# A three-stage chain on one core: the first tile's four opening hidden products, and the place of one weight subtraction

## The chip, the cores and the metric

One NeuronCore of a Trainium2 chip runs the whole program. The metric is the time of one execution on the device, in microseconds (us), taken as the median of several runs. The engines are named as in the profile: PE (TensorE, matrix products), PEld (its weight loads), DVE (VectorE), ACT (ScalarE), POOL (GpSimd), SP (SyncE, which here only issues DMAs).

## The reference

```python
X = np.fft.fft(x, axis=1); X = np.fft.fft(X, axis=2); x = X.real      # x is 4 x 3072 x 256
x_prev = x shifted by one along the sequence (a zero row first)
xk = mu_k * x + (1.0 - mu_k) * x_prev
xr = mu_r * x + (1.0 - mu_r) * x_prev
k = np.maximum(xk @ w_k, 0.0)                                         # w_k 256 x 1024
v = k * k @ w_v                                                       # w_v 1024 x 256
r = 1.0 / (1.0 + np.exp(-(xr @ w_r)))                                 # w_r 256 x 256
x = r * v
# then: top-1 routing to 8 experts of capacity 384, in order of the tokens;
# each expert: y = relu(x @ w1) @ w2, scaled by the gate's probability, back to the token's row
```

## The kernel before

Each fp32 operand of a large product is split into a high part (rounded to fp32r) and a low part (the original minus the high part), and a product is the sum of three matmuls: high by high, high by low, low by high (function product, L290 to L298). The high parts are written by ACT as copies, the low parts by DVE or POOL as subtractions, and semaphores count them.

Work is done in tiles of 512 tokens, six to a batch of 3072. For a batch, the two Fourier transforms come as matmuls (step 1, step 2, step 3) that leave the transposed result in the tile xt. The first batch's transform has nothing beside it and is written out in the functions first_dft of each engine. Its last pieces are the sums of step 3 (DVE, L920), their mirror images (ACT, L697), and an edge row that goes out and back in by DMA (L473, L475).

Then tile 0 is prepared on DVE and ACT: difference (L924) and mix (L931) give xk_raw and xr_raw for each half h of the 256 channels, high_part (ACT, L736, counted by x_high) and low_part (DVE, L937, counted by mixed) split them. The halves are xk 0, xk 1, xr 0, xr 1 in this order. The difference of half 1 waits for the edge's DMA.

The hidden layer has eight blocks f of 128 columns. An up(n, f) is six matmuls (three for each half of the channels) into the bank hb[f % 2]; ACT takes its relu (hidden, L753, counted by hb_drained), DVE squares it (L1037), ACT makes the high part (L748) and DVE the low part (L1032), and down(n, f) multiplies by w_v into the two banks vb. Eight PSUM banks exist: hb is banks 0 and 1, vb banks 2 and 3, rb (the gate's products) banks 4 and 5, and banks 6 and 7 serve the routing.

In the first tile of a batch, first_ups (L1318 to L1332) runs blocks 0 and 1 together: the high by high and low by high matmuls of half 0 of both blocks (L1327), then the high by low ones (L1330), then the same for half 1, so that PE can begin while half 1 isn't there yet. For n = 0, before(n) then issues up(0, 2) and up(0, 3) (L1370, L1371), each of which waits until ACT has taken the relu of the block that held its bank. Then come the gate's twelve matmuls (gate_in), which wait for the low parts of xr, and for wr_split in tile 0; then up 4, up 5, down 0, up 6 and so on. Up to that place PE runs four warming matmuls (keep_warm, L374) after step 3.

The weights w_k, w_r, w_v are split during the first transform: ACT makes the high parts between its other work (L713, L715, L717) and POOL subtracts in this order: four pieces of wk (L601), wr (L603), then casts half of wv (L605), four quarters of wv (L608), and two small casts and a copy for the routing (L610 to L612). DVE's own order in first_dft is: pairs and outputs of step 1, outputs of step 2 (even_out, L911, L912), sums of step 3 (L920), difference and mix of tile 0.

The order of each engine's work is written out by hand; the functions walk, before, after and rest go through the tiles. Tiles go on until every expert is full, which the kernel reads at run time.

Of the kernel before, what the change touches and what calls it, by code (L numbers as in the profile page):

```python
# [18 lines left out]
P = 128  # L19
# [25 lines left out]
TILES = SEQ // TOK  # L45
# [8 lines left out]
CREDIT = 2  # L54
# [41 lines left out]
def build(nc, ins, out, cap):  # L96
# [104 lines left out]
    hb = banks[0:2]  # L201
# [166 lines left out]

    edge_bank = banks[6]

    def keep_warm_with(count, stationary, moving, bank=lb):

        for _ in range(count):
            done = nc.tensor.matmul(bank[0:stationary.shape[-1], 0:moving.shape[-1]], stationary, moving, start=True, stop=True)  # L374
        return done
# [84 lines left out]
    with ctx:  # L460
        with nc.Block("main") as block:
# [129 lines left out]
            @block.gpsimd  # L591
            def _(pool):
                nc.gpsimd.memset(warm[:, :], 0.0).then_inc(setup, 1)
                nc.gpsimd.memset(blank[:, 0:ROW - 1], 0.0).then_inc(setup, 1)
                nc.gpsimd.memset(blank[:, ROW - 1:ROW], FAR).then_inc(setup, 1)
                nc.gpsimd.memset(full[:, 0:2], 0).then_inc(routed, 2)
                pool.sem_inc(rows_free, 1)
                nc.gpsimd.memset(padded[:, :, :], 0.0)
                for i, (h, cols) in enumerate(WK_PIECES):
                    pool.wait_ge(wk_high, i + 1)  # L600
                    nc.gpsimd.tensor_tensor(wk[:, 1, h, cols], raw_wk[:, h, cols], wk[:, 0, h, cols].bitcast(fp32), ALU.subtract).then_inc(wk_split, 1)  # L601
                pool.wait_ge(wr_high, 1)
                nc.gpsimd.tensor_tensor(wr[:, 1, :, :], raw_wr[:, :, :], wr[:, 0, :, :].bitcast(fp32), ALU.subtract).then_inc(wr_split, 1)  # L603
                pool.wait_ge(wv_in, 16)
                nc.gpsimd.tensor_copy(wv[:, 0, WV_HALVES[1], :], raw_wv[:, WV_HALVES[1], :]).then_inc(wv_high, 1)  # L605
                pool.wait_ge(wv_high, len(WV_HALVES))
                for part in WV_QUARTERS:
                    nc.gpsimd.tensor_tensor(wv[:, 1, part, :], raw_wv[:, part, :], wv[:, 0, part, :].bitcast(fp32), ALU.subtract).then_inc(wv_split, 1)  # L608
                pool.wait_ge(consts_in, 16 * CONSTS)
                nc.gpsimd.tensor_copy(earlier[:, :], small[:, 0:P])  # L610
                nc.gpsimd.tensor_copy(ones[:, :], small[:, P:2 * P])
                nc.gpsimd.tensor_copy(token[:, :], token0).then_inc(tables, 1)  # L612
                pool.wait_ge(slots_blank, 16)

                def route(m):
                    if m > 0:
                        pool.wait_ge(scattered, 16 * GRP * m)
                        pool.sem_inc(rows_free, 1)
                    pool.wait_ge(row_copied, CREDIT + GRP * (m + 1))
                    pool.wait_ge(slots_ready, m + 1)  # L620
                    if may_be_full(m):
                        pool.wait_ge(first_rows_in, 16 * needed_at(m))
                    for g in range(GRP):
                        nc.gpsimd.indirect_dma_start(  # L624
                            out=slots_dram,
                            out_offset=bass.IndirectOffsetOnAxis(ap=slot[:, g:g + 1], axis=0),
                            in_=rows[:, g, :], in_offset=None,
                            bounds_check=SLOTS - 1, oob_is_err=False,
                        ).then_inc(scattered, 16)

                def before(n):
                    if n > 0:
                        route(n - 1)

                walk(pool, before, lambda n: None, lambda: route(NTILE - 1))

                for left in (pe_left, act_left, dve_left, sp_left):
                    pool.wait_ge(left, 1)
                pool.wait_ge(w_in[0], 16)
                for half in (slice(0, FT // 2), slice(FT // 2, FT)):  # L640
                    nc.gpsimd.tensor_copy(down_w[0][:, 0, half, :], raw_down[0][:, half, :]).then_inc(down0_high, 1)
                for k, half in enumerate((slice(0, FT // 2), slice(FT // 2, FT))):
                    pool.wait_ge(down0_high, k + 1)
                    nc.gpsimd.tensor_tensor(down_w[0][:, 1, half, :], raw_down[0][:, half, :], down_w[0][:, 0, half, :].bitcast(fp32),
                                            ALU.subtract).then_inc(down0_ready, 1)
                pool.wait_ge(out_zeroed, 16 * ZEROED)
                with pool.Fori(0, EXPERTS // 2) as turn_no:
                    for i in range(2):
                        e = 2 * turn_no + i
                        for j in range(SP):  # L650
                            pool.wait_ge(ye_ready, SP + e * SP + j + 1)
                            pool.sem_inc(waits_held, 1)
                            nc.gpsimd.indirect_dma_start(  # L653
                                out=out, out_offset=bass.IndirectOffsetOnAxis(ap=who[:, i, j:j + 1], axis=0),
                                in_=ye[:, i, j, :], in_offset=None,
                                bounds_check=NTOK - 1, oob_is_err=False,
                            ).then_inc(written[i], 16)
                for i in range(2):
                    pool.wait_ge(written[i], 16 * SP * EXPERTS // 2)

            @block.scalar
            def _(act):
# [87 lines left out]
                def hidden(n, f):  # L750
                    act.wait_ge(hb_full, n * FT + f + 1)
                    act.wait_ge(square_ready, n * FT + f + 1)
                    nc.scalar.activation(relu[:, f % 2, :], hb[f % 2][:, :], ACT.Relu).then_inc(hb_drained, 1)  # L753
                    if f > 0:
                        square_high(n, f - 1)

# [117 lines left out]
            def _(dve):  # L874
# [64 lines left out]
                def first_dft():  # L939
                    pair(0, 0)  # L940
                    pair(0, 1)
                    step1_out(0, first_pairs, 0)
                    pair(0, 2)
                    step1_out(0, first_pairs, 1)
                    pair(0, 3)
                    pair(0, 4)
                    step1_out(0, first_pairs, 2)
                    step1_out(0, first_pairs, 3)
                    step1_out(0, first_pairs, 4)
                    for i in range(len(TRIPLES)):  # L950
                        even_out(0, first_pairs, i)
                    for g in range(QUADS):
                        sums(0, first_quads, g)
                    dve.wait_ge(consts_in, 16 * CONSTS)
                    dve.wait_ge(s3_summed, DH * QUADS)
                    dve.wait_ge(near_mirrored, DH * QUADS)
                    difference(0, 0, 0)
                    mix(0, 0, 0)
                    dve.wait_ge(near_edge_in, 32)
                    difference(0, 1, 0)  # L960
                    low_part(0, 0)
                    mix(0, 1, 0)
                    mix(0, 2, 0)
                    low_part(1, 0)
                    mix(0, 3, 0)
                    low_part(2, 0)
                    low_part(3, 0)
                    nc.vector.tensor_scalar(next_slot[:, :], expert_no, float(cap), None, ALU.mult)
                    nc.vector.tensor_scalar(limit[:, :], expert_no, float(cap), float(cap), ALU.mult, ALU.add)
# [240 lines left out]
            def _(pe):  # L1210
# [107 lines left out]
                def first_ups(n):  # L1318

                    for h in range(DH):  # L1320
# [8 lines left out]
                        for f in range(2):  # L1329
                            done = mm(hb[f][:, :], wk[:, 0, h, f * P:(f + 1) * P], xk[:, 1, h, :], start=False, stop=h == 1)  # L1330
                            if h == 1:
                                done.then_inc(hb_full, 1)  # L1332

                def gate_in(n, h, kh):
                    cut = slice(h * P, (h + 1) * P)
                    done = product(pe, rb[h][:, :], [(wr[:, 0, kh, cut], wr[:, 1, kh, cut], xr[:, 0, kh, :], xr[:, 1, kh, :])],
# [4 lines left out]
                def down(n, f):  # L1341
                    pe.wait_ge(squared, CREDIT + n * FT + f + 1)
                    if f == 0:
                        pe.wait_ge(x3_done, DH * (n + 1))
                        pe.wait_ge(row_copied, CREDIT + GRP * n)
                        if n == 0:
                            pe.wait_ge(wv_split, len(WV_QUARTERS))
                    for h in range(DH):
                        cut = slice(h * P, (h + 1) * P)
# [8 lines left out]

                def before(n):
                    seq, stage = n // TILES + 1, stage_of(n)  # L1360
                    if n % TILES == 0:
                        first_ups(n)
                        if n > 0:
                            route_rows(n - 1)
                    else:
                        pe.wait_ge(mixed, len(MIXED) * n + DH + 1)
                        up(n, 0)
                        route_rows(n - 1)
                        up(n, 1)
                    if n == 0:  # L1370
                        up(n, 2)  # L1371
                        up(n, 3)
                    pe.wait_ge(mixed, len(MIXED) * (n + 1) + 1)
                    pe.wait_ge(gated, DH * (n + 1))
                    if n == 0:
# [163 lines left out]
```

## Time and profile before

| | us |
|---|---|
| median of 3 runs | 614.53 |
| lowest, highest | 614.29, 615.75 |
| the profiled execution, its own time | 614.96 |
| its span (first to last instruction) | 613.2 |
| busy in it: PE, DVE, ACT, POOL | 598.6, 449.3, 316.1, 104.2 |
| mean granted TensorE clock | 0.994 |

The 1.8 us between the profiled execution's time and its span lie around the instructions. In rows of a timeline, the first number is the start in us from the beginning of the span, the second is the length of the group, then come the engine, the line, what is written and read, the shape and the count; brackets at the end give the idle time of the engine before it and what ended that.

### The profile page before, as it was taken

To read this page: it belongs to the slowest core of one execution; us is meant where nothing else is said; L and a number is where in the kernel's file an instruction comes from. 1 tells how busy PE (TensorE), PEld (TensorE's weight loads), DVE (VectorE), ACT (ScalarE), POOL (GpSimd) and SP (SyncE) were. 2 spreads that over 40 slices of the span, in tenths; PEclk is the share of its full clock that TensorE was granted. 3 is DMA by queue.
4 is the path that set the end of the run, shared out by engine and by line. 5 is a ranking of instruction groups with operands and counts; after the bars stand their busy time and mean duration, and the time that the engine had idled before them with its cause. 6 is when DMAs were issued, how large, how long until landed. Compare 5 with 4: busy or idle time off the path is not lost.

```text
span 613.2 us, 10505 instructions
## 1 busy us (share of the span) xinstructions
PE 598.6 (98%) x3358; PEld 516.0 (84%) x3358; DVE 449.3 (73%) x1053; ACT 316.1 (52%) x668; POOL 104.2 (17%) x106
## 2 busy tenths in 40 slices
PE   8989999999999999999999999999998999999995
PEld 5958888888888888888888888788887999999995
DVE  4577888877776688889786767787873777766671
ACT  1664545454546564645454545554543565664550
POOL 0720302020202011202020202020206111011111
PEclk9999999999999999999999999999998999999998
DMA  8439935151510005301010100033105834455000
GB/s 306 150 94 222 378 114 191 67 176 52 182 52 23 2 8 178 107 5 43 22 37 1 34 1 3 29 120 118 30 1 178 303 130 140 156 190 182 34 26 26
DMA packets 42157, 62.99 MB, mean 103 GB/s; under 512 B 4582, under 2 KB 32055, under 8 KB 42108
## 3 DMA queue, kind: packets, MB, share of 16 engines
q1 hardware_dynamic: 38268, 55.88, 28.3%
q0 software_dynamic: 3840, 6.52, 3.0%
q8 instruction: 23, 0.38, 0.3%
q14 instruction: 26, 0.21, 0.1%
HBM read 39.90 MB, written 26.91 MB: 109 GB/s over the span
## 4 chain that ended last, share of the span: by engine, by line
PE 92%; DVE 1%; DMA 1%; issue 1%; SPq 1%; ACT 1%; POOL 0%; POOLq 0%; ACTq 0%
PE bank L298 77%; PE bank L1295 4%; PE bank L1242 3%; PE bank L1254 2%; PE bank L1227 2%; DMA first_partner<-in_x 1%; PE bank L1465 1%; PE bank L1327 1%; PE bank L1474 1%; PE bank L1478 1%; DVE xt L920 0%; PE bank L1475 0%; SPq L468 0%; SPq L479 0%; ACT xt L697 0%
## 5 line engine op out<-in xcount | busy, mean ns | idle before, releaser
L298 PE MATMUL bank<-xk,wk 128*128 128x512 f32 x648 | 165.7, 399 | 0.9 <-ACT relu L753 0.9
L298 PE MATMUL bank<-k,wv 128*128 128x512 f32 x672 | 165.3, 396 | 0.0
L298 PEld LDWEIGHTS bank<-k,wv 128*128 128x128 f32 x672 | 125.7, 188 | 28.8
L298 PEld LDWEIGHTS bank<-xk,wk 128*128 128x128 f32 x648 | 119.8, 189 | 27.2 <-ACT relu L753 1.3
L753 ACT ACTIVATE relu<-bank 128x512 f32<-128x512 f32 x114 | 67.7, 596 | 119.3 <-PE bank L298 116.2
L624 POOL DMA_INDIRECT dispatched<-rows,slot x56 | 59.2, 1058 | 373.0 <-DVE slot L1018 323.9
L1037 DVE TENSOR_TENSOR square<-relu 128x512 f32<-128x512 f32 x113 | 77.9, 692 | 34.6 <-ACT relu L753 26.3
L1032 DVE TENSOR_TENSOR k<-square,k 128x512 fp32r<-128x512 f32 x112 | 76.9, 686 | 2.8 <-ACT k L748 2.8
L748 ACT ACTIVATE k<-square 128x512 fp32r<-128x512 f32 x113 | 70.6, 625 | 11.1 <-DVE square L1037 10.8
L298 PE MATMUL bank<-down_w,he 128*128 128x256 f32 x576 | 70.9, 284 | 0.0
L298 PEld LDWEIGHTS bank<-down_w,he 128*128 128x128 f32 x576 | 69.6, 192 | 0.0
L1198 DVE SCALAR_TENSOR_TENSOR he<-bank,he 128x384 fp32r<-128x384 f32 x64 | 35.7, 558 | 37.3 <-ACT he L866 37.3
L866 ACT ACTIVATE he<-bank 128x384 fp32r<-128x384 f32 x64 | 31.5, 492 | 57.0 <-PE bank L298 31.8
L298 PE MATMUL bank<-xr,wr 128*128 128x512 f32 x180 | 47.2, 402 | 0.0
L653 POOL DMA_INDIRECT out_rows<-ye,who x24 | 23.6, 985 | 112.9 <-DVE ye L1207 108.6
L298 PEld LDWEIGHTS bank<-xr,wr 128*128 128x128 f32 x180 | 32.8, 188 | 6.8
L1051 DVE TENSOR_TENSOR x<-gate_r,bank 128x512 f32<-128x512 f32 x28 | 19.1, 687 | 19.5 <-PE bank L298 19.5
L736 ACT ACTIVATE xr<-xr_raw 128x512 fp32r<-128x512 f32 x30 | 18.9, 631 | 22.6 <-DVE xr_raw L931 22.2
L298 PE MATMUL bank<-xe,up 128*128 128x384 f32 x168 | 29.8, 334 | 0.0
L298 PE MATMUL bank<-xe,up_high 128*128 128x384 f32 x112 | 29.4, 344 | 0.0
L298 PEld LDWEIGHTS bank<-xe,up 128*128 128x128 f32 x168 | 29.2, 188 | 0.0
L1295 PEld LDWEIGHTS bank<-fan,x 128*128 128x128 f32 x224 | 28.0, 190 | 1.2
(134 smaller groups left out, 719.6 us busy)
## 6 DMA issues: line engine op xcount, KB each, us to landing
out_rows<-blank SPq DMA_DIRECT2D x16, 768.0 KB, 4.0
raw_up<-in_moe_w SPq DMA_DIRECT2D x8, 1024.0 KB, 5.1
raw_down<-in_moe_w SPq DMA_DIRECT2D x8, 1024.0 KB, 8.6
got<-dispatched SPq DMA_DIRECT2D x16, 409.5 KB, 3.1
x_area<-in_x SPq DMA_DIRECT2D x12, 384.0 KB, 5.7
y<-in_x SPq DMA_DIRECT2D x9, 384.0 KB, 6.8
dispatched<-blank SPq DMA_DIRECT2D x1, 3276.0 KB, 20.2
first_partner<-in_x SPq DMA_DIRECT2D x3, 384.0 KB, 6.6
```

What stands on the lines that cost most here:

```text
L298: done = nc.tensor.matmul(bank, w, x, start=first and i == 0, stop=last and i == len(terms) - 1)
L624: nc.gpsimd.indirect_dma_start(out=slots_dram, out_offset=bass.IndirectOffsetOnAxis(ap=slot[:, g:g + 1], axis=0), in_=rows[:, g, :], in_of ...
L653: nc.gpsimd.indirect_dma_start(out=out, out_offset=bass.IndirectOffsetOnAxis(ap=who[:, i, j:j + 1], axis=0), in_=ye[:, i, j, :], in_offset ...
L736: nc.scalar.activation(high[:, 0, h, :], raw[:, h, :], ACT.Copy).then_inc(x_high, 1)
L748: nc.scalar.activation(k2_at(0, f), square[:, f % 2, :], ACT.Copy).then_inc(k2_high, 1)
L753: nc.scalar.activation(relu[:, f % 2, :], hb[f % 2][:, :], ACT.Relu).then_inc(hb_drained, 1)
L866: nc.scalar.activation(he[:, 0, f, :], hbe[f % 3][:, 0:cap], ACT.Relu).then_inc(he_high, 1)
L1032: nc.vector.tensor_tensor(k2_at(1, f), square[:, f % 2, :], k2_at(0, f).bitcast(fp32), ALU.subtract).then_inc(squared, 1)
L1037: nc.vector.tensor_tensor(square[:, f % 2, :], relu[:, f % 2, :], relu[:, f % 2, :], ALU.mult).then_inc(square_ready, 1)
L1051: nc.vector.tensor_tensor(x3[:, h, :], gate_r[:, h, :], vb[h][:, :], ALU.mult).then_inc(x3_done, 1)
L1198: nc.vector.scalar_tensor_tensor(he[:, 1, f, :], hbe[f % 3][:, 0:cap], 0.0, he[:, 0, f, :].bitcast(fp32), ALU.max, ALU.subtract).then_inc( ...
L1295: done = mm(tb[g][:, h * SPLIT:(h + 1) * SPLIT], x3[:, h, g * P:(g + 1) * P], fan[:, h, :], start=True, stop=True)
```

## The change

The first tile's four opening ups become one function, opening_ups, over four banks: hb[0], hb[1], vb[0], vb[1]. All matmuls on half 0 of the channels come first for the four blocks (eight with the high part of xk, four with the low part), then those on half 1 block by block. ACT's relu of blocks 2 and 3 in tile 0 reads from vb. The first down, which writes vb, waits for four relus (hb_drained). The subtraction that makes the low part of wr moves from POOL, where it stood between wk and wv, to DVE, between even_out and sums of the first transform.

```diff
@@ new names @@
+    opening_banks = hb + vb
+
+    def up_bank(n, f):
+
+        return opening_banks[f] if n == 0 and f < len(opening_banks) else hb[f % 2]
@@ POOL @@
-                pool.wait_ge(wr_high, 1)
-                nc.gpsimd.tensor_tensor(wr[:, 1, :, :], raw_wr[:, :, :], wr[:, 0, :, :].bitcast(fp32), ALU.subtract).then_inc(wr_split, 1)
@@ ACT, hidden @@
-                    nc.scalar.activation(relu[:, f % 2, :], hb[f % 2][:, :], ACT.Relu).then_inc(hb_drained, 1)
+                    nc.scalar.activation(relu[:, f % 2, :], up_bank(n, f)[:, :], ACT.Relu).then_inc(hb_drained, 1)
@@ DVE, first_dft @@
                     for i in range(len(TRIPLES)):
                         even_out(0, first_pairs, i)
+                    dve.wait_ge(wr_high, 1)
+                    nc.vector.tensor_tensor(wr[:, 1, :, :], raw_wr[:, :, :], wr[:, 0, :, :].bitcast(fp32), ALU.subtract).then_inc(wr_split, 1)
                     for g in range(QUADS):
                         sums(0, first_quads, g)
@@ PE @@
+                def opening_ups():
+
+                    blocks = [(f, bank, slice(f * P, (f + 1) * P)) for f, bank in enumerate(opening_banks)]
+                    pe.wait_ge(x_high, 1)
+                    for f, bank, cut in blocks:
+                        for part in range(2):
+                            mm(bank[:, :], wk[:, part, 0, cut], xk[:, 0, 0, :], start=part == 0, stop=False)
+                    pe.wait_ge(mixed, 2)
+                    for f, bank, cut in blocks:
+                        mm(bank[:, :], wk[:, 0, 0, cut], xk[:, 1, 0, :], start=False, stop=False)
+                    pe.wait_ge(x_high, 2)
+                    for f, bank, cut in blocks:
+                        for part in range(2):
+                            mm(bank[:, :], wk[:, part, 1, cut], xk[:, 0, 1, :], start=False, stop=False)
+                        pe.wait_ge(mixed, 3)
+                        mm(bank[:, :], wk[:, 0, 1, cut], xk[:, 1, 1, :], start=False, stop=True).then_inc(hb_full, 1)
@@ PE, down @@
                         if n == 0:
+                            pe.wait_ge(hb_drained, CREDIT + len(opening_banks))
                             pe.wait_ge(wv_split, len(WV_QUARTERS))
@@ PE, before @@
-                    if n % TILES == 0:
+                    if n == 0:
+                        opening_ups()
+                    elif n % TILES == 0:
                         first_ups(n)
-                        if n > 0:
-                            route_rows(n - 1)
+                        route_rows(n - 1)
@@
-                    if n == 0:
-                        up(n, 2)
-                        up(n, 3)
```

## Rows read from the trace of the kernel before

**Rows 1.** The page, part 1: busy time of PE, share of the span, instructions.

```profile
PE 598.6 (98%) x3358; PEld 516.0 (84%) x3358; DVE 449.3 (73%) x1053; ACT 316.1 (52%) x668; POOL 104.2 (17%) x106
```

**Rows 2.** Waits of PE over the span: total us, times, longest.

```profile
PE bank L1327 <- ACT xk L736: 1.2, 2, 0.8
PE bank L298 <- ACT relu L753: 0.9, 1, 0.9
...
PE bank L1254 <- DVE xt L920: 0.5, 2, 0.2
```

**Rows 3.** Timeline of PE, 16 to 48 us.

```profile
29.99 3.61 PE L374 MATMUL bank<-relu 128*128 128x512 f32 x8
34.43 1.17 PE L1327 MATMUL bank<-xk,wk 128*128 128x512 f32 x4 [0.84 <-ACT xk L736]
...
36.45 1.19 PE L1327 MATMUL bank<-xk,wk 128*128 128x512 f32 x4 [0.38 <-ACT xk L736]
...
39.01 3.06 PE L298 MATMUL bank<-xk,wk 128*128 128x512 f32 x12 [0.91 <-ACT relu L753]
41.91 2.96 PE L298 MATMUL bank<-xr,wr 128*128 128x512 f32 x12
44.71 2.96 PE L298 MATMUL bank<-xk,wk 128*128 128x512 f32 x12
```

**Rows 4.** Timeline of POOL, 16 to 48 us.

```profile
19.68 5.23 POOL L601 TENSOR_TENSOR wk<-raw_wk,wk 128x512 fp32r<-128x512 f32 x4 [18.41 <-ACT wk L713]
24.88 1.26 POOL L603 TENSOR_TENSOR wr<-raw_wr,wr 128x512 fp32r<-128x512 f32 x1
26.09 1.03 POOL L605 CAST wv<-raw_wv 128x1024 fp32r<-128x1024 f32 x1
27.20 4.98 POOL L608 TENSOR_TENSOR wv<-raw_wv,wv 128x512 fp32r<-128x512 f32 x4
32.12 0.76 POOL L610 CAST earlier<-small 128x128 bf16<-128x128 f32 x1
```

**Rows 5.** Timeline of DVE, 16 to 48 us.

```profile
25.75 1.22 DVE L920 TENSOR_TENSOR xt<-bank,odd_copy 128x480 f32<-128x480 f32 x2 [1.56 <-ACT odd_copy L691]
...
29.29 1.64 DVE L920 TENSOR_TENSOR xt<-bank,odd_copy 128x360 f32<-128x360 f32 x4 [0.86 <-PE bank L1254]
31.43 1.29 DVE L924 TENSOR_TENSOR xr_raw<-xt 128x512 f32<-128x512 f32 x1 [0.50 <-ACT xt L697]
32.77 0.75 DVE L931 SCALAR_TENSOR_TENSOR xk_raw<-xr_raw,mu_k,xt 128x512 f32<-128x512 f32 x1
33.78 0.69 DVE L924 TENSOR_TENSOR xr_raw<-xt 128x512 f32<-128x512 f32 x1 [0.26 <-DMA xt<-edge]
...
36.43 0.69 DVE L937 TENSOR_TENSOR xk<-xk_raw,xk 128x512 fp32r<-128x512 f32 x1
...
37.70 1.51 DVE L937 TENSOR_TENSOR xr<-xr_raw,xr 128x512 fp32r<-128x512 f32 x2
...
46.94 0.69 DVE L1037 TENSOR_TENSOR square<-relu 128x512 f32<-128x512 f32 x1 [2.73 <-ACT relu L753]
```

**Rows 6.** The line L924 on DVE: count, then ns least/median/most.

```profile
L924 DVE TENSOR_TENSOR xr_raw<-xt x30: 680/686/1295, 31.4 to 442.4; 128x512 f32<-128x512 f32 x30
```

**Rows 7.** Timeline of ACT, 16 to 48 us.

```profile
23.61 0.63 ACT L715 ACTIVATE wr<-raw_wr 128x512 fp32r<-128x512 f32 x1
...
33.55 0.63 ACT L736 ACTIVATE xk<-xk_raw 128x512 fp32r<-128x512 f32 x1 [2.31 <-DVE xk_raw L931]
...
38.39 1.05 ACT L753 ACTIVATE relu<-bank 128x512 f32<-128x512 f32 x2
```

**Rows 8.** Busy time by windows, 466 to 467 us; PEclk is the third number from the end.

```profile
466.00:467.00 1.00, 1.00 (x5) 1.00 (x4) 0.00 (x0) 0.48 (x1) 1.00 (x2) 0.50 0.87 328
```

**Rows 9.** The chain that ended last, from 400 us on: start, length, what.

```profile
466.49 8.39 PE bank L298 x42
...
485.20 7.28 PE bank L298 x42
```

## The prediction

> **What bounds the kernel now.** I read the page first. PE is busy for 598.6 us of a span of 613.2 [rows 1], so time can only come from PE's few gaps or from work taken off PE, and the change takes no matmul away: 24 matmuls stand before it and after it. The second view is the list of PE's waits. Between the first tile and the end of the span it names next to nothing: 0.5 us in two waits behind the sums of later transforms [rows 2]. Ahead of that stand two waits for ACT's high parts of xk (1.2 us) and one for a relu (0.9 us) [rows 2], all in the stretch that the change rewrites. So whatever PE gains before about 42 us it should keep to the end, provided that DVE and ACT follow it.
>
> The third view is PE's timeline of that stretch [rows 3]. The warming matmuls end at 33.60 (29.99 + 3.61). Half 0 starts at 34.43, half 1 at 36.45, blocks 2 and 3 at 39.01, the gate at 41.91. Where PE isn't held, twelve matmuls take 2.80 us (41.91 to 44.71), that is 0.233 us each. From 34.43 to 41.91 are 7.48 us for 24 matmuls that need 5.60. The 1.88 us left over are about 0.6 before half 1 (36.45 less 34.43 less 1.40), 1.16 before blocks 2 and 3 (39.01 less 36.45 less 1.40) and 0.1 at the gate.
>
> The fourth view is the other engines' timelines, for what each start waited on. Half 1 can't come before the edge's DMA: DVE's second L924 starts at 33.78 when that lands [rows 5], and PE gets its high part at 36.45 [rows 3]. The relu that holds block 2 starts at 38.39 [rows 7].
>
> **The four blocks in one.** Half 0 now offers twelve matmuls, 2.80 us, instead of six. From a start at 34.43 they would run to 37.23, and half 1 is there at 36.45: the first gap goes. Half 1's twelve follow with no relu to wait for, so the second goes too. The end is at 34.43 + 5.60 = 40.03; I add 0.1 for the slow first matmuls (the first four take 1.17 us as a group [rows 3]) and the 0.1 that stood ahead of the gate: the gate starts at 40.2, 1.7 us earlier. Its condition, the low parts of xr, is met at 39.21 (37.70 + 1.51 [rows 5]).
>
> **The subtraction leaves POOL.** POOL's L603 takes 1.26 us and starts at 24.88 [rows 4]. Everything behind it on POOL, the cast and the four wv subtractions that ended at 32.12 when L610 began [rows 4], comes forward by up to 1.2 us. Who waits for that? The first down waits for wv_split, and that comes at 47.5 (44.71 + 2.80 [rows 3]), 15 us later. But there is a hidden one. The first L924 on DVE took 1.29 us, while the median of 30 is 0.686 [rows 6]. It started at 31.43 inside POOL's last L608 and ended at 32.72, 0.60 after that one ended at 32.12 [rows 4, 5]. That is a whole subtraction run after POOL's, not beside it. POOL's L610 looks the same from its side: 0.76 us for 128 columns, where the cast of 1024 columns took 1.03 [rows 4]. So I read DVE's two-input instructions on SBUF and POOL's as taking turns. With POOL's last wv subtraction over at about 30.9, L924 takes 0.69, L931 (32.77) comes 0.6 earlier, ACT's high part (33.55 [rows 7]) too, and PE starts at 33.83 instead of 34.43; that is still behind the warming matmuls' 33.60.
>
> The Trainium skill, SBUF — State Buffer, section "Who interferes with whom", says that a DVE instruction with two SBUF inputs and a GpSimd instruction that reads SBUF exclude each other for the whole instruction, and that issue order decides who waits. By that rule the sum is the 2.3 us below; without it, with an L924 that is slow for a cause of its own, it is 1.7. The trace agrees with it in the 1.29 us.
>
> **The subtraction arrives on DVE.** Its input, ACT's L715, is there at 24.24 (23.61 + 0.63 [rows 7]). DVE is idle for 1.56 us before its first sum at 25.75, which waits for ACT's odd_copy [rows 5]. Behind the new wait on DVE stand the sums, but ACT itself does L715 before that odd_copy, so the wait adds nothing. The work is 128x512 with both inputs in SBUF, like L937's 0.69 [rows 5]. By the turns just read it is held until POOL's fourth wk subtraction ends at 24.9 [rows 4]: bounds 0.69 alone and 1.3 as in L924. I take 1.3, the nearer row: it ends near 25.5, before 25.75. Cost nothing. If that cover goes, the sums wait, and there another 0.86 us of idle (before 29.29 [rows 5]) absorbs it. In its turn it holds POOL's L605 to about 25.5, so POOL's last wv subtraction ends nearer to 31.5 than 30.9; L924 may then lose 0 to 0.1 of its 0.6.
>
> **The sum.** Start 33.83, plus 24 times 0.233 and the 0.1, gives 39.5; the gate at 39.6 instead of 41.91, so 2.3 us. On the way: half 1 is reached at 36.7 (there since 36.45), its third matmul at 37.2 (low part at 36.43 + 0.69 = 37.12 [rows 5]), the gate at 39.6 (39.21). The margins of 0.05 to 0.4 us show that the start could hardly give more. Then what follows must keep up. ACT's first relu stays at 38.39, behind the high parts of xr [rows 7]. Four relus and three high parts at the 0.5 us each that the pair of relus shows (1.05 for two) are an estimate of 42.1, with DVE's squares between. The gate now ends at 42.4, where up 4 needs only the third relu; the first down, with its new wait for the fourth, comes at 45.2. Three microseconds to spare: cost nothing, and if it were gone, PE would stand one for one. DVE had 2.73 us of idle before block 4's square [rows 5]; a PE that is 2.3 us earlier uses most of it. No later row shows PE waiting for a DMA, so nothing at a fixed time takes it back. Bounds of the gain in all: 1.7 from below for these two steps, 2.4 from above.
>
> Against the profiled execution's own 614.96 that is 612.7. The median of the runs shown is 0.43 us lower, so the median after should be 612.2.
>
> **The rivals.**
> - L924 isn't relieved: POOL is pushed back after all, or the 1.29 us have another cause. For: it is one row out of 30. Against: the two ends on POOL and DVE fit to 0.1 us. Gain 1.7: 612.8.
> - The gain is swallowed later. At 466 us, after PE's gap at the change to the experts, the granted clock is 0.50, the level of 1.2 GHz [rows 8], and 42 matmuls take 8.39 us there and 7.28 when repeated at full clock [rows 9]. That loss of 1.1 us may come twice as long or not at all once all before it moves by 2.3 us. Longer: 612.2 + 1.1 = 613.3. Not there: 611.1.
> - Slower: DVE's new subtraction doesn't get its turn at 24.9, and POOL goes on with its queue first, to 30.9. It then ends at 31.5, the eight sums (1.22, 1.22 and 1.64 back to back, 4.1 us) end at 35.6 instead of 30.9, and PE starts at 34.43 + 4.7 - 0.6 = 38.5. Gate at 44.3, 2.4 us late: 616.9. It decides from where the subtraction ends: before 26.6 it costs nothing, at 28.9 it has eaten the gain. Against: L924 got its turn at 32.12 ahead of L610, which was next on POOL [rows 4, 5].
> - The change doesn't do what it says: PE still stands before half 1 or the gate, for a part that is late after all (a slower mix, a later DMA), and 1 us or less comes off: 614.
>
> **How the numbers follow.** A measurement of this kernel can tell about 0.3% from no change, 1.84 us: faster means below 612.69. Forecast 0.60; L924 not relieved 0.16; clock stretch longer 0.08, gone 0.04; not what it says 0.07; slower by the turns 0.05. The forecast's 612.2 lies 0.5 below the bound, and medians of three differ by some tenths, so I count 0.50 of its 0.60 as faster, 0.07 of the 0.16, all of the 0.04: 0.61. Slower 0.05. Same 0.34. The range goes from 611.1 (the clock case) to 613.9 (it takes in the unrelieved L924, the longer clock stretch and most of the weak form).
>
> **What would show it.** In the changed profile: one group of eight and then four matmuls from 33.8 on, with no idle before the gate, and the gate at 39.6; no wait of PE for a relu in its list; L924's most at 0.7 to 0.8 us instead of 1.295; a DVE subtraction of wr of about 1.25 us from 24.24; the sums still at 25.75; POOL's first quarter of wv at 26.0 to 26.6. Wrong it would be if the sums start later than 25.9, if PE's first matmul stays at 34.4, or if PE waits before up 4 or the first down.

## The result, and the profile after

Medians of 22 runs each: 613.38 us after, 614.63 before. The ratio is 0.9983 with a 95% interval of 0.9977 to 0.9988, so the kernel is 0.17% faster: about 1.0 us by the ratio, 1.25 by the medians. That is real, but smaller than the 0.3% that the prediction called telling, and about half of the 2.3 us that it forecast. The profiled execution has 613.78 us, with a span of 612.0 against 613.2: 1.2 us less.

PE in the rewritten stretch, its timeline after (to be held against [rows 3]):

```profile
29.91 3.60 PE L380 MATMUL bank<-relu 128*128 128x512 f32 x8
33.74 2.10 PE L1346 MATMUL bank<-xk,wk 128*128 128x512 f32 x8 [0.23 <-ACT xk L740]
36.09 1.20 PE L1349 MATMUL bank<-xk,wk 128*128 128x512 f32 x4 [0.24 <-DVE xk L941]
37.41 0.72 PE L1353 MATMUL bank<-xk,wk 128*128 128x512 f32 x2
38.14 0.50 PE L1355 MATMUL bank<-xk,wk 128*128 128x512 f32 x1
...
40.56 2.96 PE L298 MATMUL bank<-xr,wr 128*128 128x512 f32 x12
43.37 2.96 PE L298 MATMUL bank<-xk,wk 128*128 128x512 f32 x12
```

PE starts at 33.74, as forecast (33.83). The wait for a relu is gone. But the gate starts at 40.56, not 39.6: PE waits for the low part of half 0 (36.09 instead of about 35.7), reaches half 1 at 37.41 instead of 36.7, and stands there again before its third matmul (38.14 instead of 37.2). The low part of half 0 is late too because DVE makes it only after the second difference, which is held.

DVE after, same view (to be held against [rows 5]):

```profile
24.20 1.20 DVE L957 TENSOR_TENSOR wr<-raw_wr,wr 128x512 fp32r<-128x512 f32 x1
25.67 1.22 DVE L924 TENSOR_TENSOR xt<-bank,odd_copy 128x480 f32<-128x480 f32 x2 [0.28 <-ACT odd_copy L695]
...
31.36 0.79 DVE L928 TENSOR_TENSOR xr_raw<-xt 128x512 f32<-128x512 f32 x1 [0.50 <-ACT xt L701]
32.18 0.75 DVE L935 SCALAR_TENSOR_TENSOR xk_raw<-xr_raw,mu_k,xt 128x512 f32<-128x512 f32 x1
34.73 0.69 DVE L928 TENSOR_TENSOR xr_raw<-xt 128x512 f32<-128x512 f32 x1 [1.80 <-DMA xt<-edge]
```

The moved subtraction takes 1.20 us and the sums start no later for it. The first difference takes 0.79 us instead of 1.29. All of this is as forecast. What isn't is the last row: the second difference waits 1.80 us for the edge's DMA and starts at 34.73 instead of 33.78. The chain that ended last, before and then after, has the same step:

```profile
32.12 1.63 DMA xt<-edge
```

```profile
32.05 2.66 DMA xt<-edge
```

The same 1.0 KB transfer, issued at the same time, takes 1.0 us longer. Why, the DMA view of 32 to 35 us shows; its second line is GB/s in 40 slices of 75 ns. Before, then after:

```profile
GB/s 0 0 0 0 0 0 0 0 0 14 0 0 0 0 0 0 0 0 10 3 0 0 0 0 0 0 109 0 0 0 0 0 0 0 0 0 0 0 0 0
q14 instruction: 1, 0.01, 1.0%
```

```profile
GB/s 0 0 0 0 0 0 0 0 14 0 0 0 0 0 0 0 0 10 109 0 0 0 0 0 3 0 0 0 0 0 0 0 0 0 0 0 0 0 0 0
q14 instruction: 1, 0.01, 0.9%
```

The small numbers are the edge's 16 packets, eight for each of its two DMAs; the 109 is one packet of queue q14, instructions. Its bytes are all counted in the slice where it starts, but it lasts longer: 0.9% of 16 engines over 3 us is 0.43 us. Before, that packet came at 33.95, after the edge's last (slices 18 and 19, up to 33.5). Now it comes at 33.35, in the middle of them: the last two edge packets follow only at 33.8. The same view of 33 to 34 us after, in slices of 25 ns, shows that this is just when the instruction packet ends: it starts at 33.36 (328), takes 0.45 us (2.8% of 16 engines over 1 us), and the last two edge packets come at 33.80 (the single 10).

```profile
GB/s 0 0 0 0 0 0 0 0 0 0 0 0 20 10 328 0 0 0 0 0 0 0 0 0 0 0 0 0 0 0 0 0 10 0 0 0 0 0 0 0
q14 instruction: 1, 0.01, 2.8%
```

From the gate on, nothing was lost. The last tile ended, and PE's idle time at the change to the experts began, 418.8 us after the gate's start in both (460.67 less 41.91, 459.40 less 40.56). Chain before, then after:

```profile
460.67 2.30 issue
```

```profile
459.40 2.72 issue
...
465.75 7.94 PE bank L298 x42
```

The idle time there is 0.42 longer and the slow stretch at the lower clock 0.45 shorter (7.94 against 8.39 [rows 9]). Of the 1.35 us gained at the gate, 1.2 are in the span.

### The profile page after: what moved, and what is told of

It is laid out like the page before. It is cut to its first block, busy times and chain, and to the rows that moved or that the text cites. A ratio compares the mean times of both kernels' runs of the same rounds, so it can differ in the third digit from the quotient of the medians.

```text
span 612.0 us, 10505 instructions
## 1 busy us (share of the span) xinstructions
PE 598.2 (98%) x3358; PEld 515.3 (84%) x3358; DVE 449.8 (74%) x1054; ACT 315.8 (52%) x668; POOL 103.5 (17%) x105
## 4 chain that ended last, share of the span: by engine, by line
PE 93%; DMA 2%; DVE 1%; issue 1%; SPq 1%; ACT 1%; POOL 0%; POOLq 0%; ACTq 0%
PE bank L298 77%; PE bank L1301 4%; PE bank L1248 3%; PE bank L1260 2%; PE bank L1233 2%; DMA first_partner<-in_x 1%; PE bank L1487 1%; PE bank L1333 1%; PE bank L1496 1%; PE bank L1497 1%; PE bank L1500 1%; DVE xt L924 0%; SPq L474 0%; DMA xt<-edge 0%; SPq L485 0%
## 5 line engine op out<-in xcount | busy, mean ns | idle before, releaser
L298 PE MATMUL bank<-xk,wk 128*128 128x512 f32 x636 | 162.6, 399 | 0.0
L298 PEld LDWEIGHTS bank<-xk,wk 128*128 128x128 f32 x636 | 117.5, 188 | 25.6
L1204 DVE SCALAR_TENSOR_TENSOR he<-bank,he 128x384 fp32r<-128x384 f32 x64 | 35.7, 557 | 37.1 <-ACT he L870 33.7
```

Source lines behind the costliest of these rows:

```text
L298: done = nc.tensor.matmul(bank, w, x, start=first and i == 0, stop=last and i == len(terms) - 1)
L1204: nc.vector.scalar_tensor_tensor(he[:, 1, f, :], hbe[f % 3][:, 0:cap], 0.0, he[:, 0, f, :].bitcast(fp32), ALU.max, ALU.subtract).then_inc( ...
```

## The experiments

Theory A: the instruction packet belongs to DVE's own code. It is asked for at a fixed place in that code, and the relief of the first difference brings that place 0.6 us forward, on top of the edge's DMA. Rival B: the late landing was the luck of one execution. Rival C: the four-block form delays it. Rival D: DVE has one more instruction ahead of that place, and the relief has nothing to do with it.

This table has all runs; times are in us. "Edge" is the time from the issue of the second edge DMA to the second difference on DVE; "packet" is where the q14 packet comes, counted from that same issue (negative is earlier). Each ratio is to runs of the kernel before that were made beside it (medians of 614.39 to 614.63).

| kernel | first difference | packet | edge | gate starts | median | ratio, 95% |
|---|---|---|---|---|---|---|
| before | 1.29 | 1.9 | 1.66 | 41.91 | 614.63 | 1 |
| the change | 0.79 | 1.3 | 2.68 | 40.56 | 613.38 | 0.9983 (0.9977 to 0.9988) |
| e1 ups alone | 1.29 | 2.1 | 1.66 | 39.95 | 612.77 | 0.9974 (0.9963 to 0.9985) |
| e2 subtraction alone | 0.76 | 1.3 | 2.80 | 43.04 | 615.66 | 1.0020 (1.0011 to 1.0029) |
| e3 change, DVE padded | 0.77 | -9 | 1.67 | 39.64 | 612.22 | 0.9963 (0.9950 to 0.9975) |
| e4 change, ACT padded | 0.76 | 1.3 | 2.72 | 40.50 | 613.18 | 0.9977 (0.9968 to 0.9986) |
| e5 change, POOL made late | 1.20 | 2.0 | below 2.11 | 40.69 | 613.10 | 0.9980 (0.9971 to 0.9989) |
| e6 change, DVE padded by 4 | 0.72 | 0.3 | 1.88 | 39.53 | 612.63 | 0.9971 (0.9961 to 0.9981) |
| e7 subtraction alone, DVE padded | 0.75 | -9 | 1.65 | 42.28 | 614.61 | 1.0004 (0.9995 to 1.0013) |
| e8 ups alone, DVE padded | 1.32 | -9 | 1.66 | 39.94 | 612.26 | 0.9969 (0.9958 to 0.9979) |
| e9 change, two memsets later | 0.78 | 1.7 | 1.65 | 39.15 | 612.18 | 0.9966 (0.9956 to 0.9977) |
| e10 the change again | 0.76 | 1.3 | 2.65 | 40.28 | 613.13 | 0.9979 (0.9970 to 0.9988) |
| e11 e3 again | 0.77 | -9 | 1.66 | 39.68 | 612.45 | 0.9970 (0.9960 to 0.9981) |

The gate's start also carries the input loads' differences at the very beginning: the whole of e9 is 0.4 us early and e7 0.4 us late (their first differences start at 30.96 and 31.82, not 31.4), and e10 is 0.3 us early (31.11). e6 is about 0.3 us early as well, up to the sums (the last group of them starts at 28.98, not 29.3).

**e1, one half of the change.** The wr subtraction goes back to POOL; opening_ups stays.

```diff
+                pool.wait_ge(wr_high, 1)
+                nc.gpsimd.tensor_tensor(wr[:, 1, :, :], raw_wr[:, :, :], wr[:, 0, :, :].bitcast(fp32), ALU.subtract).then_inc(wr_split, 1)
...
-                    dve.wait_ge(wr_high, 1)
-                    nc.vector.tensor_tensor(wr[:, 1, :, :], raw_wr[:, :, :], wr[:, 0, :, :].bitcast(fp32), ALU.subtract).then_inc(wr_split, 1)
```

> The four blocks in one alone; the wr subtraction stays on POOL. Theory A (an instruction packet of queue q14, which comes 0.6 us earlier once L924 is relieved, falls into the edge's DMA and delays its landing by 1 us): here L924 stays at 1.29 us, the packet stays near 33.9, the edge lands near 33.8, PE starts at 34.4 without a gap and the gate starts at 40.2: 1.7 us under the kernel before, so better than the whole change. Rival B (the late landing of 34.7 was the luck of one execution, and the rest of the 2.3 us is lost elsewhere): 1.7 us less 1, and worse than the whole change, which has L924 relieved as well. Rival C (the four-block form itself delays the landing): landing at 34.7 here too.

By the median, half of the change is 0.6 us faster than all of it: 612.77. The intervals of the two ratios overlap, so the runs alone don't settle it; the gate's start, 0.6 us earlier, points the same way. Its PE and DVE timelines:

```profile
34.30 2.10 PE L1346 MATMUL bank<-xk,wk 128*128 128x512 f32 x8 [0.74 <-ACT xk L742]
```

```profile
31.40 1.29 DVE L930 TENSOR_TENSOR xr_raw<-xt 128x512 f32<-128x512 f32 x1 [0.50 <-ACT xt L703]
...
33.75 0.69 DVE L930 TENSOR_TENSOR xr_raw<-xt 128x512 f32<-128x512 f32 x1 [0.27 <-DMA xt<-edge]
```

PE starts later (34.30) than in the whole change, and the first difference is slow again, but the edge is there at 33.75 and the gate starts at 39.95. Rivals B and C had expected otherwise.

**e2, the other half.** The kernel before, with only the subtraction moved (the DVE and POOL parts of the change's diff).

> The subtraction on DVE alone, with the old first_ups. Theory A: L924 about 0.8 us, the instruction packet near 33.3, the edge lands near 34.7, everything behind it is 0.9 us late, gate near 42.8: 0.8 to 0.9 us slower than the kernel before. Rival B: landing at 33.8 most times, no change in time to 0.2 us, since half 1 sets the path. Rival C: landing at 33.8, no change.

It is slower than before by 0.2% (1.2 us), on the DVE row that Theory A named:

```profile
34.92 0.69 DVE L922 TENSOR_TENSOR xr_raw<-xt 128x512 f32<-128x512 f32 x1 [1.95 <-DMA xt<-edge]
```

```profile
GB/s 0 0 0 0 0 0 0 0 3 11 0 0 0 0 0 0 0 0 119 0 0 0 0 0 0 0 3 0 0 0 0 0 0 0 0 0 0 0 0 0
```

Again the packet (119) sits among the edge's, and the last of these comes 0.6 us after it. The gate starts 1.13 us late. Both forms pay the landing's lateness nearly in full: the old one 1.1 us here for a landing 1.1 us late, and the four-block form 0.9 us for 1.0, by the change's gate at 40.56 against e3's 39.64 below. (The 0.6 us between the change and e1 is what is left of that when the relief of the first difference is taken off.)

**e3 and e4, whose packet it is.** 24 instructions that only count up an unused semaphore, at the head of DVE's program, and in e4 of ACT's.

```diff
+                for _ in range(24):
+                    dve.sem_inc(padding, 1)
                 dve.sem_inc(square_ready, CREDIT)
```

> The whole change with 24 semaphore instructions ahead of DVE's first load wait (DVE is idle there for 4 us). If the q14 packet is DVE's code, it moves several us earlier, the edge lands near 33.7, the gate starts at 39.6 and the time is 1.0 us under the whole change. If the packet is another engine's it stays at 33.3 and the landing at 34.7. Rival B: landing varies without regard to the packet.

> The same with the 24 instructions on ACT, ahead of its first work. If the packet is ACT's code: packet gone from 33.3, landing near 33.7, gate 39.6, 1.0 us under the whole change. If not: packet at 33.3, landing 34.7, gate 40.6. Rival B: landing varies without regard to the packet.

In e3 the packet comes at 23.0, and nothing but the edge's packets is left between 32 and 35 us; the landing is 33.8, the gate 39.64, the time 612.22, the 2.3 us that the prediction had counted. PE's rows are now the forecast's:

```profile
33.82 2.10 PE L1349 MATMUL bank<-xk,wk 128*128 128x512 f32 x8 [0.21 <-ACT xk L741]
35.76 1.09 PE L1352 MATMUL bank<-xk,wk 128*128 128x512 f32 x4
36.69 0.62 PE L1356 MATMUL bank<-xk,wk 128*128 128x512 f32 x2
...
39.64 2.95 PE L299 MATMUL bank<-xr,wr 128*128 128x512 f32 x12
```

In e4 the packet stays among the edge's, and landing and gate stay as in the change (34.67 and 40.50). So the code is DVE's.

**e5, POOL made late again.** After its wk pieces POOL subtracts wr once and a half into an unused part of gate_r.

```diff
+                pool.wait_ge(wr_high, 1)
+                nc.gpsimd.tensor_tensor(gate_r[:, 0, :].rearrange("p (h d) -> p h d", h=DH), raw_wr[:, :, :], wr[:, 0, :, :].bitcast(fp32), ALU.subtract).then_inc(wr_split, 1)
+                nc.gpsimd.tensor_tensor(gate_r[:, 1, 0:DIM], raw_wr[:, 0, :], wr[:, 0, 0, :].bitcast(fp32), ALU.subtract).then_inc(wr_split, 1)
...
-                        pe.wait_ge(wr_split, 1)
+                        pe.wait_ge(wr_split, 3)
```

> The whole change with POOL made as late as before again: after its wk pieces it subtracts wr once more into an unused part of gate_r, and half of wr a second time (1.9 us of needless POOL work). Theory A: POOL's wv subtraction that is under way at 31.4 ends near 32.1, so DVE's first difference takes about 1.3 us, DVE's instruction packet comes 0.6 us later, near 33.9, the edge lands near 33.8, PE starts at 34.3 without a gap, the gate starts at 40.0: 0.6 us FASTER than the whole change, with more work. Rival D (the packet moved because DVE has one more instruction ahead of it, not because DVE was early): packet stays near 33.3, landing 34.7, and the gate at 40.6 or later.

A miss in the time, and useful all the same. The packet did move to 34.1 and the edge was there before DVE asked for it, with DVE's number of instructions unchanged from the whole change: Rival D falls, since it had the packet stay. But POOL was later than planned, and DVE's second instruction had to wait for it too:

```profile
31.36 1.20 DVE L931 TENSOR_TENSOR xr_raw<-xt 128x512 f32<-128x512 f32 x1 [0.50 <-ACT xt L704]
32.60 1.64 DVE L938 SCALAR_TENSOR_TENSOR xk_raw<-xr_raw,mu_k,xt 128x512 f32<-128x512 f32 x1
```

```profile
28.28 5.41 POOL L615 TENSOR_TENSOR wv<-raw_wv,wv 128x512 fp32r<-128x512 f32 x4
```

So PE started at 35.04, and what the landing gave the turns took.

**e6, a small dose.** As e3, with range(4).

> As e3 with 4 semaphore instructions on DVE instead of 24. Theory A: the packet is asked for at a fixed place in DVE's code; four instructions earlier it is asked for before the sums' end, at 29 to 31 us, and comes ahead of the edge's DMA: landing 33.8, gate 39.6, 1.0 us under the whole change, as e3. If the gain of e3 has another cause (the warm-up of DVE, the long delay), 4 instructions give less.

Four instructions move the packet from 1.3 to 0.3 us after the issue, the edge takes 1.88, the gate starts at 39.53. That gate looks better than it is, since the execution is some 0.3 us early. DVE also stood 0.4 us longer before its first difference than in the other runs, and its input was no later:

```profile
31.55 0.72 DVE L931 TENSOR_TENSOR xr_raw<-xt 128x512 f32<-128x512 f32 x1 [0.92 <-ACT xt L702]
```

The chain of e6 has 0.47 us of "issue" there, time in which DVE waited for nothing that the profile shows; why, no run tells. So a small dose clears the landing but isn't a full cure. The median, 612.63, isn't told apart from e3's by the intervals.

**e7 and e8, each half with the packet out of the way.** e2 and e1 with e3's 24 instructions.

> The subtraction on DVE with the old first_ups, and e3's 24 semaphore instructions on DVE. Theory A: landing 33.8 again, first difference 0.8 us, and half 1 sets the path, so the time is that of the kernel before to 0.2 us: the relief of POOL's turn alone is worth nothing with the old ups, and the 1.2 us that e2 lost come back. Otherwise it stays at 615.6.

> The four blocks in one with the subtraction on POOL, and the 24 semaphore instructions on DVE. Theory A: the packet wasn't in the way in e1, so no change from e1: 612.8, gate at 40.0, and 0.5 us above e3: that is what the relief of L924 is worth when the packet is out of the way. If the padding gains here too, by over 0.3 us, it does something else than move the packet.

e7 is the kernel before again, 1.0004: with the old ups, the relief of the first difference gives nothing, and all that e2 lost was the packet. e8 has e1's gate (39.94 and 39.95), as expected. Its median is 0.5 lower than e1's (0.3 by the ratios), more than the 0.3 that was allowed for; the intervals overlap, the first tile is the same, and what makes it stays open. Beside e3 (39.64, 612.22) e8 (39.94, 612.26) shows what the relief is worth with the packet gone: 0.3 to 0.4 us at the gate (e8's first difference also starts 0.1 earlier), too little to see in the medians.

**e9, the same cure without an added instruction.** Two of DVE's early memsets go behind the low parts of the first tile.

```diff
-                nc.vector.memset(need[:, :], 16.0 * GRP)
-                nc.vector.memset(base[:, :], 0.0).then_inc(route_step, 1)
...
                     low_part(3, 0)
+                    nc.vector.memset(need[:, :], 16.0 * GRP)
+                    nc.vector.memset(base[:, :], 0.0).then_inc(route_step, 1)
                     nc.vector.tensor_scalar(next_slot[:, :], expert_no, float(cap), None, ALU.mult)
```

> The whole change with two of DVE's early memsets (need, base) moved behind the first tile's low parts, so DVE has two instructions less ahead of the place where it asks for its next code. Theory A: the packet is asked for at a fixed place in DVE's code, two instructions further on, where DVE stands until the edge is there; it comes after 34 us, the edge lands near 33.8, the gate starts at 39.6 and the time is 612.2 to 612.6, with no instruction added. If the gain of e3 and e6 came from the padding itself, the landing stays at 34.7 and the time at 613.4.

> The whole change once more, beside e9 and e11 on one chip. Theory A: packet near 33.3, landing near 34.7, gate 40.6, 613.2 to 613.4, as before. Rival B (luck of one execution): the landing is elsewhere.

> e3 once more, with more rounds, beside e10 on one chip. Theory A: packet near 23, landing near 33.8, gate 39.6, 0.9 to 1.1 us under e10.

612.18 for e9, beside 613.13 for the change itself on the same chip: 0.95 us under it, and not to be told apart from e3's 612.22. The packet comes 0.3 us behind the last edge packet, at 33.3 and not after 34 us as expected (the whole execution and its landing are 0.4 to 0.5 us early), and that is enough:

```profile
GB/s 0 0 7 7 0 0 0 0 0 0 0 0 10 3 0 0 0 109 0 0 0 0 0 0 0 0 0 0 0 0 0 0 0 0 0 0 0 0 0 0
```

```profile
33.31 0.69 DVE L926 TENSOR_TENSOR xr_raw<-xt 128x512 f32<-128x512 f32 x1 [0.79 <-DMA xt<-edge]
```

e10 repeats the change's late landing (2.65) and e11 the padded one's early one (1.66), which closes Rival B: in eight profiles with the packet before 1 us or after 1.5 us from the issue and DVE waiting for the edge, it is there after 1.65 to 1.88; in four with the packet at 1.3, after 2.65 to 2.80. e11's median is 0.7 us under e10's, a little less than the 0.9 to 1.1 expected.

## Why the prediction was wrong where it was

- **What bounds the kernel.** Right: the time came from PE's gaps before 42 us, and all that was gained at the gate stayed to the end but 0.15 us. The slow stretch after the change to the experts grew no longer, which was a rival at 0.08. The list of PE's waits after has no relu.
- **The four blocks in one.** Right in mechanism; the size was 1.7 and the gate starts 1.96 us earlier when it stands alone (e1, 41.91 to 39.95). Its start was 0.13 earlier, and of the two times 0.1 that I added only about 0.05 was needed (39.95 less 34.30 is 5.65). By the ratio it gives 1.6 us (0.9974).
- **The subtraction leaves POOL.** Right that DVE and POOL take turns and that the first difference comes down to 0.7 to 0.8: 0.79. POOL's rows after say it from its side:

```profile
24.77 1.52 POOL L609 CAST wv<-raw_wv 128x1024 fp32r<-128x1024 f32 x1
...
31.32 0.28 POOL L614 CAST earlier<-small 128x128 bf16<-128x128 f32 x1
31.55 0.75 POOL L615 CAST ones<-small 128x128 bf16<-128x128 f32 x1
```

The cast of 1024 columns grows from 1.03 to 1.52 where DVE's subtraction was waiting ahead of it, and the 128-column cast falls from 0.76 to 0.28 where DVE isn't in its way. What I mis-sized is what the 0.6 us are worth: 0.3 to 0.4 at the gate, since half 1 then binds (in e3 its third matmul waits until 37.21).
- **The step that failed** is the sentence "Half 1 can't come before the edge's DMA: DVE's second L924 starts at 33.78 when that lands", and its use in the sum: "half 1 is reached at 36.7 (there since 36.45)". I took the landing as fixed, and looked for a DMA at a fixed time only in later rows. But a DVE that is 0.6 us early has its next code fetched 0.6 us early (33.95, then 33.35), and that packet meets the edge's: landing 34.71, gate 40.56. With the packet elsewhere, the sum holds to 0.1 us (e3: 33.82 and 39.64 for 33.83 and 39.6). The relief, counted as 0.6 us gained, was a net loss: the ups alone have the gate at 39.95.
- **The subtraction arrives on DVE.** Right: 1.20 us from 24.20, sums not delayed. The slower rival with POOL going first didn't come. The rival "a part that is late after all (a slower mix, a later DMA)" is the one that happened, at the chance of 0.07, with 1.35 us left and not 1.
- **The numbers.** 613.38 lies inside the range of 611.1 to 613.9, 1.2 above the forecast, and on the "same" side of the 0.3%. That it lies inside is partly luck: the upper end was drawn mainly for an unrelieved L924 and a longer clock stretch, neither of which came, and the rival that did come was priced at 614, just outside, though the range was meant to take in most of it.

The Trainium skill, Runtime: NRT & Kernel Launch, section "Instruction fetch mechanics", says that each sequencer fetches its next block of code by DMA while it runs the current one, and that this is mostly hidden. These runs agree with a fetch by position in the code: four instructions more ahead of it bring the packet 1.0 us earlier (e6), two fewer 0.4 us later (e9). They add that the packet, itself hidden, can cost 1.0 us through a small transfer that it meets.

## What to carry to other kernels

Where a DMA of a few small packets is on the critical path, don't take its latency as fixed (here it was 1.65 to 2.80 us): look in the DMA view for instruction packets near it, and remember that a change in DVE's pace (e5) or in the number of its instructions (e3, e6, e9) moved them here. Measure the halves of a change apart even when both are plausible: here one half alone did at least as well as both. A few instructions moved across the critical wait (two memsets) bring back what such a meeting costs. But as few as two to four instructions moved the packet by 0.4 to 1.0 us, so such a cure has to be looked at again after each edit.

## What I had not expected of the hardware

One q14 packet of 0.01 MB put 1.0 to 1.1 us on another DMA of 1.0 KB when it came 1.3 us after that DMA's issue; at 0.3 us after it cost 0.2, at 1.7 nothing. About half of that can be read off: in the change's profile the packet takes 0.45 us, and the last two edge packets come 0.45 us after its start, just when it ends; the other three late profiles (e2, e4, e10) show the same with 0.5 to 0.6 us. It looks as if they stood behind it on one DMA engine, but the views don't name the engine, so that is inferred. The other half is open: the landing was counted 0.9 us after those last packets, where it had been 0.3 us before, and why the count comes so late no run here shows.
